# An attention and mixture-of-experts kernel: first expert's weights split during attention, row list without weights, first chunk turned tile by tile

## The reference

```python
# 1. clustered attention, 2 batches x 8 heads x 768 x 64: a query sees the keys of its own cluster (16)
mask = q_assign[:, :, :, None] == k_assign[:, :, None, :]
attn = softmax(where(mask, q @ k.T / 8, -1e9));  x = attn @ v          # -> [1536, 512]
# 2. noisy top-2 of 8 experts
noisy = x @ w_gate + log1p(exp(x @ w_noise)) * noise
top2, weights = two largest of noisy per token, softmax over the two
for e in range(8): out[mask_e] += weight * (relu(x[mask_e] @ w1[e]) @ w2[e])   # w1 512x1024, w2 1024x512
# 3. soft mixture: 32 slots, 4 per expert
d = softmax over tokens of x @ phi; slots = d.T @ x; slots through 8 experts; out = softmax over slots @ slot_out
```

## Time and profile before

| | |
|---|---|
| median of 3 runs | 759.21 us (758.95 to 759.32) |
| the profiled execution | 763.77 us, span 762.0 us |
| busy over the span | PE 667.5 us (88%), DVE 380.2 (50%), ACT 330.5 (43%), POOL 231.9 (30%) |
| attention | 0 to 287.9 us |
| routing | 288.6 to 313.6 us |
| experts | 313.9 to about 667 us |
| soft mixture | about 667 to 762 us |
| zeros written to y_sums by POOL's queue | 13 x 256 KB, from 15.76 us |

### The profile page before, as it was taken

How to read it: one execution, slowest core, us unless ns; L and a number is a source line. 1 busy time by engine, 2 the same in 40 slices (tenths; PEclk the granted TensorE clock), 3 DMA queues, 4 the chain that set the end, 5 groups by cost and what they waited for, 6 DMA issues and landing times. The chain is left out here.

```text
span 762.0 us, 10785 instructions
## 1 busy us (share of the span) xinstructions
PE 667.5 (88%) x4032; PEld 545.8 (72%) x4032; DVE 380.2 (50%) x626; ACT 330.5 (43%) x591; POOL 231.9 (30%) x306
## 2 busy tenths in 40 slices
PE   3899999999999991379999999999999999376977
PEld 2776766767677761379999999999999996242322
DVE  4676786867678656644435353535343431023202
ACT  5576766667576645013434343525353431021001
POOL 8855537173552000440322314140505051100000
PEclk9999999999999995669999999999999999767987
DMA  8401230302214003153463627281909099496984
GB/s 191 174 1 36 49 83 1 84 22 63 53 31 151 2 22 131 34 157 137 152 159 130 181 106 206 72 240 39 273 6 302 3 319 347 131 367 240 357 305 165
DMA packets 71138, 105.23 MB, mean 138 GB/s; under 512 B 30968, under 2 KB 39160, under 8 KB 70704
## 3 DMA queue, kind: packets, MB, share of 16 engines
q1 hardware_dynamic: 62336, 86.17, 33.9%
q0 software_dynamic: 8752, 18.38, 10.3%
HBM read 87.54 MB, written 16.99 MB: 137 GB/s over the span
## 5 line engine op out<-in xcount | busy, mean ns | idle before, releaser
L870 POOL DMA_INDIRECT y_sums<-y_rows,give x32 | 52.0, 1625 | 211.2 <-ACT y_rows L963 169.5
L443 DVE TENSOR_REDUCE row_max<-psum_a 128x1 f32<-128x768 f32 x96 | 91.6, 954 | 48.1 <-PE psum_a L537 47.6
L357 ACT ACTIVATE probs<-psum_a,row_max 128x768 f32<-128x768 f32 x96 | 86.6, 902 | 34.6 <-DVE row_max L443 33.8
L537 PE MATMUL psum_a<-w_parts 96*128 96x384 f32 (+1 forms) x384 | 94.1, 368 | 3.1 <-DVE w_parts L421 3.0
L888 PE MATMUL psum_c<-x_hi,w_parts 128*128 128x416 f32 x256 | 91.8, 359 | 1.2 <-DVE x_lo L1007 1.2
L890 PE MATMUL psum_c<-x_lo,w_parts 128*128 128x416 f32 x256 | 91.1, 356 | 0.0
L889 PE MATMUL psum_c<-x_hi,w_parts 128*128 128x416 f32 x256 | 90.8, 355 | 0.0
L1402 DVE TENSOR_TENSOR w_parts<-w_plain,w_parts 128x2048 fp32r<-128x2048 f32 x32 | 73.1, 2289 | 33.0 <-ACT w_parts L1398 32.6
L1023 DVE SCALAR_TENSOR_TENSOR h_lo<-psum_c,h_hi 128x416 fp32r<-128x416 f32 x64 | 37.8, 590 | 97.3 <-ACT h_hi L973 79.4
L547 PE MATMUL psum_a<-ident,probs 128*128 128x128 f32 x576 | 81.6, 275 | 2.4 <-DVE p_t L447 2.1
L888 PE MATMUL psum_c<-h_hi,w_parts 128*128 128x416 f32 x224 | 79.9, 357 | 0.0
(11 more groups left out here) (215 smaller groups left out, 999.1 us busy)
## 6 DMA issues: line engine op xcount, KB each, us to landing
w_plain<-in_moe_w SPq DMA_DIRECT2D x32, 1024.0 KB
w_plain<-in_moe_w SPq DMA_DIRECT2D x14, 2048.0 KB, 19.9
soft_slot<-in_moe_w SPq DMA_DIRECT2D x2, 2048.0 KB, 24.8
y_sums<-zeros POOLq DMA_DIRECT2D x13, 256.0 KB, 4.4
early_room<-in_q SPq DMA_DIRECT2D x16, 192.0 KB, 3.9
early_room<-in_k SPq DMA_DIRECT2D x16, 192.0 KB, 4.0
early_room<-in_v SPq DMA_DIRECT2D x16, 192.0 KB, 2.5
x_rows<-x_all SPq DMA_DIRECT2D x8, 384.0 KB, 3.5
```

Of the source, the lines that this page charges most:

```text
L357: nc.scalar.activation(probs[step % RING][:, :, :], sc[step % 2], ACT.Exp, bias=row_max[:, step % 4:step % 4 + 1], accum_out=den[:, step % ...
L443: nc.vector.tensor_reduce(row_max[:, step % 4:step % 4 + 1], sc[step % 2], AX.XY, ALU.max, negate=True).then_inc(max_done, 1)
L537: last = nc.tensor.matmul(sc[step % 2][:, c, :], a[par][:, h, t * P:(t + 1) * P], b[par][:, h, c * HALF * P:(c + 1) * HALF * P], start=(i ...
```

## The change

- The x_all ring has 4 slots, with a semaphore each. In the room gained, and with more of its own, attention keeps the split q and k outside the first expert's raw weights and outside quarters 0 and 1 of their high part (`own_parts`, `later`).
- SP loads all four quarters (4 MB) after the gate's matrices, ahead of unit 2.
- In the last unit ScalarE rounds quarters 0 and 1 in 8 pieces of 512 columns, one at the end of each of steps 0 to 7; VectorE subtracts them at the end of steps 2 to 9.
- Routing: three short memsets beside ScalarE's softplus instead of two long ones; no copy of chosen; thresholds that start at 0 and so need no added one; the copies of the counts after the groups; one pick and one sum for both choices; col_hot per choice; groups with the row number's product alone; the list has 60 columns instead of 120, and its weights aren't copied here.
- Experts: GpSimd's first instructions are the four gathers, straight from the list, with a semaphore each; the register loads come after. VectorE multiplies col_hot by the weights, twice 720 columns, and TensorE sums them in 48 passes to the list of weights; VectorE waits for that and copies it ahead of its first column. The first chunk is turned tile by tile into four banks, each tile after its own gather. The first block waits for each column of x by itself. Quarters 2 and 3 are cut as before.

The core of the diff:

```diff
-        q_both, k_high = [part(0), part(1)], [part(2), part(3)]
-        q_clus, k_clus = [part(4, KR), part(5, KR)], [part(6, KR), part(7, KR)]
+        own_parts = sb("own_parts", [P, 6, 2 * TW], F32R)
+        part = lambda i, rows=P: own_parts[0:rows, i, :].rearrange("p (h n) -> p h n", h=2)
+        later = lambda i: shared.parts[:, 0, 2 * shared.quarter + i * 2 * TW:2 * shared.quarter + (i + 1) * 2 * TW].rearrange("p (h n) -> p h n", h=2)
+        q_both, k_high = [later(0), part(0)], [later(1), part(1)]
+        q_clus, k_clus = [part(2, KR), part(3, KR)], [part(4, KR), part(5, KR)]
...
+                sp.dma_start(rows, x_all[:, unit % s.XRING, :, :]).then_inc(shared.x_stored[unit % s.XRING], 16)
...
+            for q in range(4):
+                shared.load_quarter(sp, w1, w2, 0, q)
             for unit in range(2, s.UNITS):
                 sp.wait_ge(prep_done, (unit - 2) * N_SLOT + 4)
                 load_raw(unit)
                 sp.wait_ge(pv_done, 2 * (unit - 2) + 2)
                 load_v(unit)
                 store_x(unit - 2)
-            for q in (2, 3):
-                shared.load_quarter(sp, w1, w2, 0, q)
             for unit in range(s.UNITS - 2, s.UNITS):
...
+                if unit + 1 == s.UNITS and n < 2 * shared.PIECES:
+                    shared.piece_to_hi(act, n)
...
+                    ring = group // 2 % s.XRING
+                    if t0 == 0 and group // 2 >= s.XRING:
+                        dve.wait_ge(shared.x_stored[ring], 16 * (group // 2 // s.XRING))
...
+                if unit + 1 == s.UNITS and 2 <= n < 2 + 2 * shared.PIECES:
+                    shared.piece_to_lo(dve, n - 2)
...
-            for q in (0, 1):
-                shared.load_quarter(sp, w1, w2, 0, q)
-            sp.wait_ge(shared.x_stored, 16 * s.UNITS)
+            for j in range(s.XRING):
+                sp.wait_ge(shared.x_stored[j], 16 * (s.UNITS // s.XRING))
...
-                last = nc.tensor.matmul(lists_ps, left[:, m, :], right[:, m, :, :].rearrange("p a c -> p (a c)"),
+                last = nc.tensor.matmul(lists_ps, left[:, m, :], right[:, m, :],
...
-            for q in (3, 0, 1):
-                shared.cut_hi(act, 0, q)
+            shared.cut_hi(act, 0, 3)
...
+            for j in range(3):
+                ins = v.memset(run[j][:, 0:8, :], 0.0)
+            step(ins)
...
-            for j in range(2):
-                v.memset(run[j][:, :, :], 0.0)
-            step(v.tensor_tensor(chosen[:, :, :], oh[0][:, :, :], oh[1][:, :, :], ALU.add))
-            step(v.tensor_copy(run[0][:, 8:, :], chosen[:, :, :]))
+            step(v.tensor_tensor(chosen, oh[:, 0, :, :], oh[:, 1, :, :], ALU.add))
-                a, b = run[j % 2], run[(j + 1) % 2]
+                a, b = run[(0, 1, 2, 1)[j]], run[(1, 2, 1, 2)[j]]
...
-            step(v.tensor_tensor(ccmp[:, :, :], n_e[:, :].rearrange("p (a c) -> p a c", c=1).to_broadcast([P, E, s.STEPS]),
-                                 thr.to_broadcast([P, E, s.STEPS]), ALU.is_gt))
+            step(v.tensor_tensor(ccmp[:, :, :], n_e[:, :].rearrange("p (a c) -> p a c", c=1).to_broadcast([P, E, s.STEPS + 1]),
+                                 thr.to_broadcast([P, E, s.STEPS + 1]), ALU.is_ge))
-            step(v.tensor_scalar(tiles[:, :], tiles[:, :], 1.0, None, ALU.add))
...
-            v.tensor_copy(shared.counts[:, 0, :], tiles[0:1, :])
-            v.tensor_copy(shared.counts[:, 1, :], offs[0:1, :])
...
-            for j in range(2):
-                step(v.tensor_tensor(pick[:, :, :], rank[:, :, :], oh[j][:, :, :], ALU.mult))
-                step(v.tensor_reduce(place[:, j, :], pick[:, :, :], AX.X, ALU.add))
+            step(v.tensor_tensor(pick[:, :, :, :], rank[:, :, :].rearrange("p (j t) e -> p j t e", j=1).to_broadcast([P, 2, NT, E]), oh[:, :, :, :], ALU.mult))
+            step(v.tensor_reduce(place[:, :, :], pick[:, :, :, :], AX.X, ALU.add))
...
+            v.tensor_tensor(value[:, 0, :, :], k["token"][:, :, :].rearrange("p b t -> p (b t)").rearrange("p (j t) -> p j t", j=1).to_broadcast([P, 2, NT]),
+                            part_of[:, :, :], ALU.subtract)
             for j in range(2):
-                ins = v.tensor_tensor(value[:, 0, j, :], k["token"][:, :, :].rearrange("p b t -> p (b t)"), part_of[:, j, :], ALU.subtract)
-            step(v.tensor_tensor(col_hot[:, :, :, :].rearrange("p j t c -> p (j t) c"),
-                                 k["cols"][:, :].rearrange("p (a c) -> p a c", a=1).to_broadcast([P, 2 * NT, s.COLS]),
-                                 both(col).rearrange("p (a c) -> p a c", c=1).to_broadcast([P, 2 * NT, s.COLS]), ALU.is_equal))
-            for m in range(0, 2 * NT, GROUP):
-                j, t = m // NT, m % NT
-                some = slice(t, t + GROUP)
-                v.tensor_tensor(left[:, m:m + GROUP, :], k["places"][:, 0:s.TILE].rearrange("p (a n) -> p a n", a=1).to_broadcast([P, GROUP, s.TILE]),
-                                part_of[:, j, some].rearrange("p (t n) -> p t n", n=1).to_broadcast([P, GROUP, s.TILE]), ALU.is_equal)
-                for a in range(2):
-                    ins = v.tensor_tensor(right[:, m:m + GROUP, a, :],
-                                          value[:, a, j, some].rearrange("p (t c) -> p t c", c=1).to_broadcast([P, GROUP, s.COLS]),
-                                          col_hot[:, j, some, :], ALU.mult)
-                ins.then_inc(right_ready, 1)
+                step(v.tensor_tensor(col_hot[:, j * NT:(j + 1) * NT, :],
+                                     k["cols"][:, :].rearrange("p (a c) -> p a c", a=1).to_broadcast([P, NT, s.COLS]),
+                                     col[:, j, :].rearrange("p (a c) -> p a c", c=1).to_broadcast([P, NT, s.COLS]), ALU.is_equal))
+                for t in range(0, NT, GROUP):
+                    some, m = slice(t, t + GROUP), j * NT + t
+                    v.tensor_tensor(left[:, m:m + GROUP, :], k["places"][:, 0:s.TILE].rearrange("p (a n) -> p a n", a=1).to_broadcast([P, GROUP, s.TILE]),
+                                    part_of[:, j, some].rearrange("p (t n) -> p t n", n=1).to_broadcast([P, GROUP, s.TILE]), ALU.is_equal)
+                    v.tensor_tensor(right[:, m:m + GROUP, :], value[:, 0, j, some].rearrange("p (t c) -> p t c", c=1).to_broadcast([P, GROUP, s.COLS]),
+                                    col_hot[:, m:m + GROUP, :], ALU.mult).then_inc(right_ready, 1)
+            v.tensor_copy(shared.counts[:, 0, :], tiles[0:1, :])
+            v.tensor_copy(shared.counts[:, 1, :], offs[0:1, :])
             dve.wait_ge(lists_done, 1)
-            v.tensor_scalar(shared.list_rows[0:s.TILE, 0:s.COLS], lists_ps[:, 0:s.COLS], k["dummy_f"][0:s.TILE, 0:1], None, ALU.add)
-            v.tensor_copy(shared.list_weights[0:s.TILE, :], lists_ps[:, s.COLS:2 * s.COLS])
+            v.tensor_scalar(shared.list_rows[0:s.TILE, 0:s.COLS], lists_ps, k["dummy_f"][0:s.TILE, 0:1], None, ALU.add)
...
+        x_first = [psum[:, 2 + c, 0:N] for c in range(KC)]
+        weights_ps = psum[0:TL, 7, 0:s.COLS]
...
+            def gather(at, t):
+                nc.gpsimd.indirect_dma_start(out=rows[:, t, :], out_offset=None, in_=dram["x"],
+                                             in_offset=bass.IndirectOffsetOnAxis(ap=at[0:TL, t:t + 1], axis=0)).then_inc(gathered[t], 16)
+            for t in range(TT):
+                gather(list_rows, t)
             regs = registers(pool, "pool")
             n, off = chunk_range(pool, regs, E - 1)
             total = off + n
-            nc.gpsimd.tensor_copy(take[:, :], list_rows[0:TL, 0:TT]).then_inc(idx_ready, 1)
-            pool.wait_ge(idx_ready, 1)
-            for t in range(TT):
-                gather(t).then_inc(gathered, 16)
...
-                pool.wait_ge(gathered, g * GATHER + GATHER)
-                pool.sem_inc(waits_over, 1)
+                for t in range(TT):
+                    pool.wait_ge(gathered[t], g * 16 + 16)
+                    pool.sem_inc(waits_over, 1)
...
+            def rows_in(g):
+                for t in range(TT):
+                    pe.wait_ge(gathered[t], g * 16 + 16)
...
-            pe.wait_ge(gathered, GATHER)
-            for c in range(KC):
-                turn_x(0, c)
+            for m in range(PAIRS):
+                if m % NT == 0:
+                    pe.wait_ge(right_ok, m // NT + 1)
+                last = nc.tensor.matmul(weights_ps, left[:, m, :], col_hot[:, m, :], start=(m == 0), stop=(m == PAIRS - 1))
+            last.then_inc(weights_done, 1)
+            for t in range(TT):
+                pe.wait_ge(gathered[t], 16)
+                for c in range(KC):
+                    last = nc.tensor.transpose(x_first[c][:, t * TL:(t + 1) * TL], rows[:, t, c * P:(c + 1) * P], k["ident"][0:TL, 0:TL])
+                    if t == TT - 1:
+                        last.then_inc(x_turned, 1)
...
-                    pe.wait_ge(x_lo_ok, g * KC + KC)
...
+                            if f == 0:
```

(27 more changed lines are left out.)

93 lines of the change are left out of this document (52 added, 41 removed).

## The result

Over 18 runs of each on one chip the changed kernel takes 758.10 us (755.13 to 762.48), the kernel before 762.67 (758.46 to 767.27). The ratio is 0.995, interval 0.9926 to 0.9974: faster by 0.5%. By the ratio that is 3.8 us (2.0 to 5.6), by the two medians 4.6, where the forecast had 10.4. The kernel before had a median of 759.21 us over the three runs that the forecast started from and has 762.67 over these 18; so 3.5 of the 9.3 us between the forecast's 748.8 and the measured 758.10 are the starting point, and 5.8 are gain that did not come.

What follows compares the result with a forecast made beforehand. TensorE paced the last attention unit, dependent VectorE instructions routing, and four gathers the hand-over. -2.5 (pieces included) - 4.15 - 3.7 = -10.35, say -10.4 us: 753.4 as profiled, 748.8 median; range 746.8 to 756.6, its own 747.4 to 751.8.

Steps and rivals of the forecast that it cites:

- first rival: Routing and hand-over: the clock stays at 1.2 GHz through both lists; gain 4.4 us, 754.8 us; chance 0.31.
- Early load: Kernel start: four 1 MB loads ahead of unit 2's q and k are through by about 42 us; cost 0.
- Pieces: Last attention unit: 16 weight pieces on ScalarE and VectorE fall mostly into holes; +0.6 us, bounds 0 and 9.7.
- The rival of 9.7 us: Last attention unit: no hole absorbs the weight pieces, +9.7 us instead of +0.6, 757.9 us; chance 0.1.
- Fewer operations: Routing: fewer VectorE operations save 1.3 us, col_hot in halves 0.8, one product less 0.26; first list matmul at 304.1 us.
- The step that failed: Routing's row list: clock returns 4.3 us after its start, list ends at 310.7 instead of 313.05; -2.5 us there.
- The prediction's own bound for no return: Routing's row list: if the clock never returns, 48 passes of 0.175 take 8.4 us; the -2.5 us becomes -0.5.
- Its second effect, "free": Experts' start: the weights' list at 2.4 GHz ends about 5.3 us in, under gathers landing at about 7.9; cost 0.
- Hand-over: Routing to experts: first gather, no longer held up by VectorE's cuts, ends 315.25 against 319.40; -4.15 us, bounds -2.8 and -4.6.
- First chunk by tile: Experts' first chunk: after the last landing, first product at +1.6 instead of +5.1, third block +8.5; -3.7 us, bounds -4.0, -2.2.

Runs made afterwards that it cites:

- The wide variants: The changed kernel with 120 instead of 60 moving columns in both lists, 753.20 us (ratio 0.9879), or in the row list only, 754.78 us (0.989).
- the variants whose clock or list was out of the way: The changed kernel with both lists wide, only the row list wide, no weights' list, or one list of 120 columns: ratios 0.9879, 0.989, 0.9885, 0.9886.

## Why the prediction was wrong

The sign was right, and the case that came is its first rival, the clock at 1.2 GHz through both lists: it had 4.4 us for it and a chance of 0.31; 3.8 were measured. That closeness is in part luck: its 6.0 us of loss up to the third block were 5.0 in the profiles, and the interval goes from 2.0 to 5.6. The forecast itself was wrong. By its own steps:

**Early load: 0.** Right. Unit 2's q and k landed in time: the profile shows no pause of TensorE for them at 50.43 us, where it turns them (50.62 in the earlier trace rows); SP had issued them by 36.3 us, and the last unit's first row maximum starts at 249.17 us (249.35 before).

**Pieces, +0.6.** Right: 0.55 us, the difference that twelve profiles show in the last unit. Attention's end by itself would not have told it, as it moves by up to 2.3 us between profiles of kernels with the same attention (285.8 to 288.1). The rival of 9.7 us is out.

**Fewer operations.** Right. The first pass of the list comes 17.04 us after attention's end where it came 19.27 after it: 2.23 us less, 2.36 forecast. That it stands at 304.04 us, forecast at 304.1, is in part chance. Pick and sum together take 0.78 us, and a group comes every 0.65.

**The step that failed: "The clock came back 3.5 us after the list began ... I take 4.3".** (In finer stretches the three returns that it read, 3.5, 5.7 and 2.8 us, are 3.8, 5.9 and 3.0; that is not what failed.) It took a return that all stretches of the trace showed under wide passes and gave it to narrow ones, on the ground that TensorE was never idle in them. It never came: 8.58 us at 1.2 GHz instead of 6.6. The prediction's own bound for no return, 8.4 us, was close. The list is ready 25.7 us after attention's end, where 23.4 had been forecast. The wide variants show the cause by its removal, the kernel before with 60 columns by its being put in alone.

**Its second effect, "free".** The weights' list was costed at nothing because at 2.4 GHz it lies under the gathers. At 1.2 GHz it took 8.58 us, ran past the last landing, and put all 16 transposes behind it. From gather to first product: 11.2 us against 8.2 forecast. Without the list 8.3, with the clock up 8.2: 2.9 us. The row list's 2.3 us, 0.4 of the first gather and 3.0 of the first product, less 0.7 behind it, are the 5.0 us by which the third block is later than forecast (45.8 against 40.8).

**Hand-over, -4.15.** Right in its mechanism, 3.7 us in the table. The first gather took 1.18 us and ended at 315.20, 0.98 behind the end of VectorE's first product, near the late end of the bounds. By the rule of the Trainium skill (SBUF — State Buffer, "SBUF: two separate sides") that of a VectorE instruction with two SBUF inputs and a GpSimd one that reads SBUF the first to start holds a shared pair of ports to its end and the other waits, a gather waits so; the 1.10 and 2.85 us without and with cuts beside it agree. Its other half, that gathers hold up VectorE's cuts, doesn't show: the two cuts at 327.72 us took 4.48 together while the gather beside them took 3.03. In the kernel before a gather (330.73 us, 1.04 long) even started ahead of the cut at 330.97, which took its usual 2.28. The wait was GpSimd's alone.

**First chunk by tile, -3.7.** In the variants whose clock or list was out of the way it gave what was said, a first product 8.2 us behind the gather instead of 11.7. In the changed kernel 0.5 of it was left. From first product to third block the changed kernel needs 6.4 us, where 7.1 was forecast. The clock returned 3.5 us behind its first product, so that h_lo, done at 332.70 us, ends the wait and not the products: VectorE was through with its four columns 1.4 us behind the first product, and 4.48 for the cuts and 0.58 for h_lo follow. The pause for h_lo is there as said, up to 0.4 us. One reading was off by a product: the prediction puts the third block before at 338.25 us, which is the 24th product; the 25th starts at 338.44. By that its part would have been -3.9 and its forecast from first product to third block 6.9.

**The size of the rest.** From the third block on the two profiles take 423.6 and 422.4 us, nearly the same. Up to it, from attention's end, the change gained 6.1 us, and 5.5 with the pieces' 0.55 taken off. The ratio gives 3.8, 2.0 to 5.6; so the profiles' gain lies just inside the interval, and of the 1.7 us between the two it can't be said whether they are more than noise. For the ten other kernels the same sum (51.8 less the third block's column, less 0.55 where there are pieces) lies inside the interval too.

## What to carry to other kernels

A clock that fell in an idle stretch has to be won back by what comes next, and TensorE being busy without a break wasn't enough for it here: look in the trace at the shape of the passes under which it rose, and don't expect it from narrower ones. Halving the moving side of a chain of small fp32 matmuls may make it longer. Before costing new work at nothing "under the gathers", put it there at both clocks; and where an instruction waits only because something long stands beside it, say where the long one goes: behind the gathers it gained nothing, in the holes of the stage before it gained 4.6 us (by the ratios of the changed kernel with and without).
